# Attention windows woven into five visits of the first expert's loop in place of seven

## The reference, cut to what matters

```
for t in range(S):
    cur = einsum('bhd,bhe->bhde', u * k[t], v[t])
    y[:, :, t] = einsum('bhd,bhde->bhe', r[t], state + cur)
    state = w[t][..., None] * state + einsum('bhd,bhe->bhde', k[t], v[t])
x = y, transposed to (3072 tokens, 384 channels)
h = x @ w_in                       # 384 -> 2048
x = piecewise(h) @ w_out           # 0 below -1, h above 1, (h + 1)**2 / 4 between
out = (silu(x @ w_gate) * (x @ w_val)) @ w_out2   # 384 -> 1536 -> 384
```

## Time and profile before

| | |
|---|---|
| median of 3 runs | 976.07 us (975.66 to 976.07) |
| profiled execution, its own time | 976.21 us |
| its span, first to last instruction | 974.3 us |
| TensorE (PE) busy | 958.0 us |
| VectorE (DVE) busy | 517.8 us |
| ScalarE (ACT) busy | 401.5 us |
| GpSimd (POOL) busy | 163.4 us |

### The profile page before, as it was taken

One profiled execution on the slowest core, in us unless ns is written; L12 is line 12 of the kernel. 1 busy time (PEld: TensorE's weight loads), 2 busy tenths in 40 slices (PEclk: granted clock), 3 DMA queues, 4 the chain that ended last, 5 costly groups with the idle time before them and its releaser, 6 DMA issues.

```text
span 974.3 us, 17480 instructions
## 1 busy us (share of the span) xinstructions
PE 958.0 (98%) x6886; PEld 940.0 (96%) x6886; DVE 517.8 (53%) x906; ACT 401.5 (41%) x841; POOL 163.4 (17%) x155
## 2 busy tenths in 40 slices
PE   6999999999999999999999999999999999999998
PEld 5899999999999999999999999999999999999997
DVE  7996766667576575764444433444333343334332
ACT  5675455455554554544675322222222222222222
POOL 6992210301102112020263200000000000000000
PEclk9999999999999999999999999999999999999999
DMA  9724212121222213100433101010100001010000
GB/s 298 244 69 140 81 61 87 54 87 52 89 78 63 88 44 97 66 5 1 130 106 98 58 7 43 1 50 1 49 0 27 22 0 48 0 48 0 25 1 26
DMA packets 23492, 59.52 MB, mean 61 GB/s; under 512 B 2688, under 2 KB 12032, under 8 KB 23424
## 3 DMA queue, kind: packets, MB, share of 16 engines
q1 hardware_dynamic: 23424, 58.59, 19.2%
HBM read 49.14 MB, written 9.44 MB: 60 GB/s over the span
## 4 chain that ended last, share of the span: by engine, by line
PE 96%; DVE 1%; DMA 1%; issue 1%; ACT 0%; SPq 0%; DVEq 0%; ACTq 0%
PE bank L1207 50%; PE bank L1235 36%; PE bank L1263 2%; PE bank L1285 2%; PE bank L1280 2%; PE bank L1255 1%; PE bank L1291 1%; PE bank L1272 1%; DMA w_by_channel<-in_w_channel 1%; DVE suf L968 0%; PE bank L1252 0%; DVE glo L1058 0%; DVE gate L1065 0%; DVE w_by_channel L978 0%; DVE k_r_by_channel L993 0%
## 5 line engine op out<-in xcount | busy, mean ns | idle before, releaser
L809 ACT ACTIVATE ghi<-gate 128x384 fp32r<-128x384 f32 x224 | 117.2, 523 | 187.6 <-DVE gate L1077 95.6
L1058 DVE TENSOR_TENSOR glo<-gate,ghi 128x384 fp32r<-128x384 f32 x224 | 133.1, 594 | 112.5 <-ACT ghi L809 110.3
L1075 DVE TENSOR_TENSOR gate<-bank,gate 128x384 f32<-128x384 f32 x96 | 53.5, 558 | 214.8 <-ACT gate L928 214.8
L1207 PE MATMUL bank<-xhi,w2gv_ahi 128*128 128x384 f32 x480 | 161.3, 336 | 0.0
L1207 PE MATMUL bank<-xlo,w2gv_ahi 128*128 128x384 f32 x480 | 161.3, 336 | 0.0
L1207 PE MATMUL bank<-xhi,w2gv_alo 128*128 128x384 f32 x480 | 161.3, 336 | 0.0
L928 ACT ACTIVATE gate<-bank 128x384 f32<-128x384 f32 x96 | 47.2, 492 | 227.5 <-PE bank L1207 227.5
L1235 PE MATMUL bank<-ghi,w1ohi 128*128 128x384 f32 x384 | 133.8, 349 | 0.9 <-DVE glo L1058 0.9
L1207 PE MATMUL bank<-xhi,w1ihi 128*128 128x384 f32 x384 | 129.2, 336 | 1.4 <-issue 0.8
L1235 PE MATMUL bank<-glo,w1ohi 128*128 128x384 f32 x384 | 129.1, 336 | 0.0
L1207 PE MATMUL bank<-xhi,w1ilo 128*128 128x384 f32 x384 | 129.1, 336 | 0.0
(11 more groups left out here) (95 smaller groups left out, 1582.4 us busy)
## 6 DMA issues: line engine op xcount, KB each, us to landing
r_k_v_by_token<-in_rkv_token SPq DMA_DIRECT2D x24, 576.0 KB, 5.0
k_r_by_channel<-in_kr_channel SPq DMA_DIRECT2D x24, 448.0 KB, 4.1
w_by_channel<-in_w_channel SPq DMA_DIRECT2D x24, 226.2 KB, 2.7
x_t<-ring SPq DMA_DIRECT2D x8, 576.0 KB, 3.0
x_raw<-x_t SPq DMA_DIRECT2D x8, 576.0 KB, 3.9
ring<-in_w_out SPq DMA_DIRECT2D x22, 192.0 KB, 2.6
out_t<-ring SPq DMA_DIRECT2D x7, 576.0 KB, 3.0
ring<-in_w_gate SPq DMA_DIRECT2D x12, 192.0 KB, 2.4
```

The lines of the kernel that those rows point to most:

```text
L809: e.activation(ghi[j % 2][:, :], gate[j % 2][:, :], ACT.Copy).then_inc(M["hi", ph], 1)
L1058: e.tensor_tensor(glo[j % 2][:, :], gate[j % 2][:, :], ghi[j % 2][:, :].bitcast(F32), ALU.subtract)\
L1075: e.tensor_tensor(q, hid[j % 2][:, 0:T], q, ALU.mult).then_inc(M["t", 2], 1)
L1207: m = e.matmul(out, w_of(a, k), x_of(b_, k), start=start and i == 0, stop=stop and i == total - 1)
```

## The change

Two pairs of visits become one each. KT and AT of window w stand ahead of Y and ST of window w - 1 in one visit. The visits are in slots 3, 6, 9, 11 and 12 in place of 3, 5, 6, 8, 9, 11 and 12; in round 0 in 4, 7, 10, 12 and 13 in place of 4, 6, 7, 9, 10, 12 and 13. The state for window w + 1 is decayed behind the drain of ST(w); it was decayed ahead of the copies of AT(w + 1). The number of fills, and each fill's matmuls, stay as they are; since the order of the fills changes, so does which fill had a bank before another.

```diff
--- before.py
+++ after.py
@@ -53,11 +53,9 @@
 
 
 VISITS = [[("KT", 0, 0), ("AT", 0, 0), ("AT", 0, 1)],
-          [("Y", 0, 0), ("ST", 0, 0), ("KT", 1, 0)],
-          [("AT", 1, 0), ("AT", 1, 1), ("XT", 0, 0)],
-          [("Y", 1, 0), ("ST", 1, 0), ("KT", 2, 0)],
-          [("AT", 2, 0), ("AT", 2, 1), ("XT", 1, 0)],
-          [("Y", 2, 0), ("ST", 2, 0)],
+          [("KT", 1, 0), ("AT", 1, 0), ("AT", 1, 1), ("Y", 0, 0), ("ST", 0, 0)],
+          [("KT", 2, 0), ("AT", 2, 0), ("AT", 2, 1), ("Y", 1, 0), ("ST", 1, 0), ("XT", 0, 0)],
+          [("Y", 2, 0), ("ST", 2, 0), ("XT", 1, 0)],
           [("XT", 2, 0)]]
 FILLS = [f for visit in VISITS for f in visit]
 NF = len(FILLS)
@@ -82,8 +80,8 @@
     return {j: tuple(FILLS.index(f) for f in visit) for j, visit in zip(slots, VISITS)}
 
 
-WIN_SLOTS = visits_at((3, 5, 6, 8, 9, 11, 12))
-WIN_FIRST = visits_at((4, 6, 7, 9, 10, 12, 13))
+WIN_SLOTS = visits_at((3, 6, 9, 11, 12))
+WIN_FIRST = visits_at((4, 7, 10, 12, 13))
 XT_FIRST = 13
 
 CHECK_SLOTS = {9: 0, 10: 1, 12: 2}
@@ -1022,7 +1020,7 @@
                 kind, w, n = fills(g)[f]
                 src = bank_of(g, f)
                 if kind == "AT":
-                    if n == 0:
+                    if n == 0 and w == 0:
                         decay_state(g, w, parity)
                     if first(g):
                         e.wait_ge(ld["cst"], 16)
@@ -1044,6 +1042,8 @@
                         rows, pairs = slice(r0, r0 + D), slice(0, n_pair)
                         ps = src[rows, 0:n_pair * D].rearrange("p (a c) -> p a c", a=n_pair)
                         e.tensor_tensor(st[rows, pairs, :], ps, sbar[twin(g, w)][rows, pairs, c0:c0 + D], ALU.add).then_inc(st_out, 1)
+                    if w < NW - 1:
+                        decay_state(g, w + 1, parity)
                 elif kind == "Y":
                     e.wait_ge(fill, g * NF + (f + 1))
                     e.wait_ge(diag_v, g * NW + w + 1)
```

## The result

The changed kernel takes 979.15 us (median of 6 runs, 978.88 to 980.99) against 976.2 for the kernel before on the same chips: ratio 1.0035, 95% interval 1.0025 to 1.0046. It is slower by 0.35%, 3 us. The forecast was 979.5.

What follows compares the result with a forecast made beforehand. It took TensorE, busy 98% of the span, as the bound. Round 0 +2.7, rounds 1 to 6 +0.4 and +0.3 for one-sided bounds gave +3.4 us on 976.07: 979.5 us, range 976.3 to 982.3.

Steps and rivals of the forecast that it cites:

- Term 1: Visits of each round: fewer switches between kinds of matmul on TensorE save 0.33 us a round, 2.3 over seven rounds.
- Term 2: Merged visits: Y waits 0.2 us for ScalarE's k_token copy; less the switching saved, +0.4 us for rounds 1 to 6.
- Term 3: Round 0, slot 7: Y waits 2.4 us and ST 1.2 behind lagging engines; round 0 in all +2.7 us.
- The bound of 0.9: Round 0: DVE's lo, moved beside another POOL subtraction, could lengthen that one, at +0.9 us.
- Rival D: Round 0, 61 to 66 us: TensorE's idle waits lower its clock; a 6 us stretch makes +3, 982.5 us; chance 0.07.
- the allowance: In the sum: +0.3 us added since the bounds of joints and latency reach further up than down.
- Rival A: All rounds: other engines follow TensorE, so drains come in time; faster, 973.0 us; chance 0.08.
- Rival B: Round 0: waits about half as long, as DVE without slot 6's two drains is ahead; 977.5 us; chance 0.2.
- Rival C: Steady rounds: KT wait is 0.4 us and ST also waits for AT's copy; +7.5, 983.6 us; chance 0.1.

Runs made afterwards that it cites:

- the second experiment: Changed kernel with rounds 1 to 6 put back to the earlier seven visits, so only round 0 keeps the change: 979.55 us, ratio 1.0041.

## Why the prediction was right, point by point

**Term 1, switching.** Forecast 0.33 us a round. With the waits taken out it is 0.31 and 0.37 in rounds 1 and 2. The joints that no row showed were taken rightly: AT to Y 1.09, ST to XT 0.56. The Trainium skill, "TensorEngine Tiling (Array Packing)", Key Properties, has the TensorE drained at each change of tiling mode; counted by that alone the saving would have been 0.2 a round (one change of 0.10 less, twice), and the measured 0.31 to 0.37 go by the rows, with the joints around KT and XT that the rule leaves out.

**Term 2, the wait for k_token.** Forecast 0.2 a visit, measured 0.16: the start follows the end of the copy by 0.05, not by the 0.10 taken from another pair of engines. So rounds 1 to 6 came out level (rounds 1 and 2 by 0.02 and 0.05 us better than before), not 0.07 worse; the 0.4 us of the sum for them, and the 0.3 added for one-sided bounds, were not there. ST and XT came behind their copies, as worked out.

**Term 3, round 0.** Forecast 2.4 and 1.2 us of waits and +2.7 in all. With a full clock the waits are 2.27 and 1.21, and round 0 takes 92.90 - 48.87 = 44.03 in the second experiment: +2.83. This term was the whole result. DVE's lo did move beside another POOL operation, but POOL's product ended 0.03 earlier than before, not 0.9 later: lo started at 62.02, in the middle of POOL's subtraction of 61.78, and took 1.17 while that took 1.00. POOL's product behind it took 1.33 in place of 1.01. The Trainium skill, "SBUF — State Buffer", says in its section on two separate sides that the first to start keeps the shared port for its whole instruction; these rows agree with that. The bound of 0.9 was too wide for another reason as well: the POOL operation of 1.93 in the earlier trace rows (56.84) stood beside a scan of w on DVE (L968, from 56.40 for 1.57), not beside a lo.

**Rival D, the clock,** had 0.07. Its mechanism did occur, at another price: 0.4 us in round 0 of the profiled execution, not 3, because the lower clock fell on matmuls that had a wait behind them. Two of the six timed runs, 980.63 and 980.99 us, lie 1.2 to 2.1 us above the other four; they too have a mean clock of 0.997, but where it was low in them isn't shown. The forecast of 979.5 is thus nearer than its parts, and that is luck: term 2 and the allowance together were about 0.9 too high, the clock was left out and round 0 was 0.1 too low, so that +3.4 stood against a measured +2.95.

**Rival A** failed where it was said to: in round 0 the other engines lag and don't follow. **Rival B** failed for the reason given, DVE's drains of slot 6 stood behind the knee that ScalarE waited for. **Rival C** needed a wait ahead of ST in the steady rounds; there is none in after.

What the prediction didn't see is that the two waits of slot 7 stand in one line: what ends the visit is DVE's copy of AT behind POOL's product, and the wait for k_token, though twice as long, costs nothing by itself: without it the visit lasts 7.67 us in place of 7.69.

## What to carry to other kernels

Merging bursts on the engine that binds saves the joints between them (here 0.33 us a round), but it also puts a producer and the reuse of its buffer into one burst; work out for each fill when the buffer it takes has been drained, from the start of the burst, and move the drain ahead of whatever stands before it in its engine's queue. Do this for the first round by itself: where other engines lag behind, a burst that comes earlier only waits longer. And a wait that is removed gives nothing as long as a later one in the same line stands: try them together before you call either harmless.

## What the runs showed of the hardware

TensorE's granted clock went from 2.4 to 1.2 GHz for 3.4 us after an idle stretch of 2.3 us, and in another kernel after one of 3.5 us. With the same 2.3 and 1.2 us of waits it stayed up in one profiled execution and, by the mean, in three of eleven timed runs, that one among them; what decides between them isn't shown. In the profiles the price hung on what the low stretch met: 0.4 us where a wait followed, 1.7 us where products did. Filling the gap with matmuls that change nothing kept the clock up in all six runs. The Trainium skill, "TensorE: Matmul & The Clock Gate", Why this matters for your kernels, advises against long idle gaps between bursts of matmuls. These runs agree that a gap can bring the clock down, but the 2.3 us here is shorter than the gaps that it warns of; the measurement decides.
